# Bucketed attention and two expert layers on one core: where GpSimd's low parts and weight splits and the first head's turn stand in their queues

## What is computed

```python
q_bits = (np.einsum('bhsd,dk->bhsk', q, proj) > 0)      # k_bits alike; bucket = sum(bits * 2**i)
scores = np.where(mask, q @ k.T / sqrt(D), -1e9)
attn = np.exp(scores - max); attn = attn / (sum(attn) + 1e-9)
x = (attn @ v)                                          # 1536 x 512 after the heads are joined
h = x @ w_in1;  g = max(h, 0) + alpha * min(h, 0);      x = g @ w_out1
h = x @ w_in2;  g = P(h) / (Q(|h|) + 1e-6);             out = g @ w_out2
```

## Time and profile before

| what | us |
|---|---|
| median of the 3 runs timed | 798.24 (794.5, 798.24, 799.77) |
| the profiled execution, its own time | 799.15 |
| its span, first to last instruction | 797.3 |
| PE busy in it | 775.7 |
| DVE, ACT, POOL busy | 517.8, 358.3, 304.9 |

### The profile page before, as it was taken

The page is one execution under the profiler, slowest core; times in us unless marked ns, Lnnn a source line. Parts: engine busy times, 40 slices in busy tenths (PEclk is TensorE's granted clock), DMA queues, the critical chain, the costliest instruction groups (busy, mean ns, idle before and its releaser), DMA issues.

```text
span 797.3 us, 11723 instructions
## 1 busy us (share of the span) xinstructions
PE 775.7 (97%) x3820; PEld 583.7 (73%) x3820; DVE 517.8 (65%) x806; ACT 358.3 (45%) x588; POOL 304.9 (38%) x357
## 2 busy tenths in 40 slices
PE   8889999999989999999999999999999999999998
PEld 5456565666656778888888888887888888888886
DVE  6776676776751654435333533379888988888886
ACT  7434554555544311112011210167766767676673
POOL 7566776776856689200000177781000000000000
PEclk9999999999999999999999999999999999999999
DMA  4666675675571243000000033330000100000001
GB/s 127 169 153 161 165 199 151 165 203 150 139 187 48 78 139 122 28 1 1 0 1 14 1 106 93 92 93 1 2 0 1 53 0 1 1 27 27 1 1 53
DMA packets 34207, 58.86 MB, mean 74 GB/s; under 512 B 9900, under 2 KB 13780, under 8 KB 34164
## 3 DMA queue, kind: packets, MB, share of 16 engines
q1 hardware_dynamic: 31796, 53.15, 24.3%
q10 hardware_dynamic: 2368, 5.15, 2.6%
HBM read 29.59 MB, written 3.24 MB: 41 GB/s over the span
## 4 chain that ended last, share of the span: by engine, by line
PE 75%; POOL 8%; issue 4%; DVE 4%; SPq 3%; DMA 3%; ACT 1%; POOLq 0%; DVEq 0%; ACTq 0%
PE acc L1375 31%; PE ps_h L1343 31%; PE ps_o L590 3%; PE ps_a L505 2%; PE ps_s L560 2%; PE ps_s L565 2%; POOL lo L866 1%; PE ps_o L612 1%; POOL p_sum L873 1%; DMA work<-rden_scratch 1%; POOL pen L882 1%; DMA q<-stats 1%; PE ps_a L501 1%; POOL x_lo L964 1%; DMA raw<-in_qk 1%
## 5 line engine op out<-in xcount | busy, mean ns | idle before, releaser
L1408 ACT ACTIVATE g_hi<-num 128x512 fp32r<-128x512 f32 x96 | 59.9, 624 | 207.2 <-PE acc L1375 203.1
L1478 DVE TENSOR_TENSOR g_lo<-num,g_hi 128x512 fp32r<-128x512 f32 x96 | 71.7, 747 | 78.2 <-ACT g_hi L1408 77.7
L1040 DVE TENSOR_REDUCE row_max<-ps_a 128x1 f32<-128x384 f32 x180 | 92.1, 553 | 40.0 <-PE ps_a L505 37.6
L736 ACT ACTIVATE p<-ps_s 128x768 f32<-128x768 f32 x96 | 77.5, 810 | 67.7 <-PE ps_s L565 64.2
L1343 PE MATMUL ps_h<-x_hi,w_late_in_hi 128*128 128x512 f32 x288 | 78.9, 395 | 1.2 <-POOL w_late_in_lo L1307 1.2
L1343 PE MATMUL ps_h<-x_hi,w_late_in_lo 128*128 128x512 f32 x288 | 78.8, 394 | 0.0
L1343 PE MATMUL ps_h<-x_lo,w_late_in_hi 128*128 128x512 f32 x288 | 78.8, 394 | 0.0
L590 PE MATMUL ps_o<-p,v_use 128*64 128x384 f32 x384 | 74.4, 507 | 0.0
L1486 DVE TENSOR_SCALAR num<-ps_h,alpha_sb 128x512 f32<-128x512 f32 x48 | 36.0, 750 | 54.4 <-PE ps_h L1343 53.7
L1416 ACT ACTIVATE den_q<-ps_h,abs_b 128x512 f32<-128x512 f32 x48 | 33.0, 688 | 83.8 <-PE ps_h L1343 77.6
L1343 PEld LDWEIGHTS ps_h<-x_hi,w_late_in_hi 128*128 128x128 f32 x288 | 53.9, 187 | 14.0 <-POOL w_late_in_lo L1307 1.7
(11 more groups left out here) (167 smaller groups left out, 1569.9 us busy)
## 6 DMA issues: line engine op xcount, KB each, us to landing
stage<-in_w_in SPq DMA_DIRECT2D x26, 256.0 KB, 2.7
stage<-in_w_out SPq DMA_DIRECT2D x26, 256.0 KB, 2.7
raw<-in_qk SPq DMA_DIRECT2D x15, 384.0 KB, 3.0
q<-hi SPq DMA_DIRECT2D x30, 192.0 KB
k<-hi SPq DMA_DIRECT2D x30, 192.0 KB
v_raw<-in_v SPq DMA_DIRECT2D x16, 192.0 KB, 3.0
work<-rden_scratch SPq DMA_DIRECT2D x16, 192.0 KB, 3.3
out<-y SPq DMA_DIRECT2D x12, 256.0 KB, 2.5
```

Source lines behind the costliest of these rows:

```text
L736: nc.scalar.activation(halves(p[c][:]), ps_s[c % 2][:, :, 0:HALF], ACT.Exp, scale=float(D) ** -0.5).then_inc(s_exp, 1)
L1040: dve.tensor_reduce(row_max[slot][:, i, c:c + 1], ps_a[:, i, 0:HALF], AX.X, ALU.max).then_inc(s_a_free, 1)
L1408: nc.scalar.activation(g_hi[f % 2][:], num[f % 4][:], ACT.Copy).then_inc(s_ghi, 1)
L1478: dve.tensor_tensor(g_lo[f % 2][:], num[f % 4][:], g_hi[f % 2][:], ALU.subtract).then_inc(s_glo, 1)
```

## The change

Six moves; no instruction is added to or taken from the work. (1) `uses_of`: in the first head the sign products of head 3 ("bits") go behind the turn of head 1 ("m"). (2) PE: the first scores of head 1, which stood ahead of the last row-maximum products and values of chunk 4 of head 0, go behind those values. (3) ACT: in head 0 the high part of head 3 is made in step 3 and no longer in step 4. (4) POOL: `x_low` leaves the end of pairs 1 to 5 and stands behind `row_stats` of the following pair's u = 0; for that, POOL's program writes out pair 1 ahead of its hardware loop. (5) POOL: the weight splits of chunks 0 and 1 go behind the penalty rows and behind `split_qk`. (6) SP: the load of weight chunk 2 (`stage_early(2)`) goes from pair 6's u = 0, where it stood ahead of the row sums' spreading, to its u = 1, behind the low parts.

```diff
--- before.py
+++ after.py
@@ -277,8 +277,8 @@
                 if first_head:
                     return [([("a", 1, 1)], [("a", 1, 2)]),
                             ([("a", 1, 3)], [("a", 1, 4)]),
-                            ([("a", 1, 5)], [("bits", 3, 0)]),
-                            ([("m", 1, 0)], [("a", 2, 0)]),
+                            ([("a", 1, 5)], []),
+                            ([("m", 1, 0)], [("bits", 3, 0), ("a", 2, 0)]),
                             ([("a", 2, 1)], [("a", 2, 2)]),
                             ([("a", 2, 3)], [("a", 2, 4)])]
                 if second_head:
@@ -352,10 +352,11 @@
 
                 return u
 
-            def over_pairs(eng, body):
-
-                body(0, 2)
-                with eng.Fori(1, PAIRS - 2) as j:
+            def over_pairs(eng, body, begin=1):
+
+                for j in range(begin):
+                    body(j, 2)
+                with eng.Fori(begin, PAIRS - 2) as j:
                     body(j, 2)
                 body(PAIRS - 2, 1)
                 body(PAIRS - 1, 0)
@@ -476,10 +477,10 @@
                             fill_b_lo(u, j + 1)
                         if first:
                             stage_early(u)
-                        if left == 1 and u == 0:
-                            stage_early(2)
                         if u == 0 and not first:
                             spread(sp, j - 1)
+                        if left == 1 and u == 1:
+                            stage_early(2)
                         if not left and u == 0:
                             stage_early(3)
 
@@ -665,7 +666,7 @@
                                 t = KC * h + c
                                 if c + 2 < KC:
                                     scores(u, j, c + 2, t + 2)
-                                elif not (final and u == 1):
+                                elif not (final and u == 1 or first and c == 4):
                                     scores(1 - u, j + u, c + 2 - KC, t + 2)
                                 for kind, g, cc in steps[c][0]:
                                     at = (u + g) % 2, j + (u + g) // 2
@@ -685,6 +686,9 @@
                                 due_sums = False
                             for c in range(begin, begin + group):
                                 values(u, h, c, KC * h + c)
+                                if first and c == 4:
+
+                                    scores(1, 0, 0, c + 2)
                             for c in range(begin, begin + group):
                                 for kind, g, cc in steps[c][1]:
                                     at = (u + g) % 2, j + (u + g) // 2
@@ -835,7 +839,7 @@
                                 sums_of(1 - u, j - 1 + u, h - 1)
                             if c == 1 and first and u == 1:
                                 stat_rows(0, 1)
-                            if c == (4 if first and u == 0 else 2) and (left > 1 or (left == 1 and u == 0)):
+                            if c == (3 if first and u == 0 else 2) and (left > 1 or (left == 1 and u == 0)):
                                 split_qk(1 - u, j + 1 + u)
                             if c == (4 if first and u == 0 else 3) and (left > 1 or (left == 1 and u == 0)):
                                 fill_a_hi(1 - u, h + 3)
@@ -990,14 +994,10 @@
                             if not (isinstance(h, int) and h == 0):
                                 v_partial(1 - u, j + u)
                             row_stats(1 - u, h + 1)
-                        if final and u == 0:
+                        if u == 0 and not (isinstance(j, int) and j < 2):
                             x_low(j - 2)
                         if not (first and u == 0):
                             add(1, h)
-                        if first and u == 1:
-                            split_weights(0)
-                        if left == 1 and u == 0:
-                            split_weights(1)
                         if final:
                             split_weights(2 + u)
                         if left > 1 or (left == 1 and u == 0):
@@ -1008,14 +1008,16 @@
                             split_qk(1 - u, j + 1 + u)
                         if first and u == 0:
                             add(1, h)
-                        if u == 1 and left > 1 and not first:
-                            x_low(j - 1)
+                        if first and u == 1:
+                            split_weights(0)
+                        if left == 1 and u == 0:
+                            split_weights(1)
                         if final and u == 0:
                             normalise(j - 1)
                         if final and u == 1:
                             x_low(j - 1)
 
-                over_pairs(pool, pair)
+                over_pairs(pool, pair, 2)
 
             def attention_vector(dve):
                 dve.memset(mcols[1][:, 0:STAT_ROW].bitcast(F32), 0.0)
```

## The result

The changed kernel takes 790.8 us (median of 7 runs, 789.68 to 792.74), the kernel before 798.26 us beside it (794.5 to 799.77); the ratio is 0.9922, 95% interval 0.9901 to 0.9943. So it is faster by 0.8%: 7.5 us between the medians and 6.2 us by the ratio; 5.4 us were forecast. The two profiled executions, 799.15 and 790.8 us, lie 8.35 us apart. Lines have moved: the turn was L516 and is L517, the row-maxima product L505 and L506, POOL's p_sum L873 and L877.

What follows compares the result with a forecast made beforehand. PE, busy 775.7 of 797.3 us, bounds the kernel; only idle and low-clock time can be won. 3.9 + 1.2 + 0 + 1.7 + 1.5 - 1.4 = 6.9, less 1.5, gives 5.4 us: 798.4 to 793.0, range 790.3 to 796.2.

Steps and rivals of the forecast that it cites:

- (c): Turns in u = 0 of pairs 2 to 6: five waits for POOL go; gain 3.86 us, bounds 2.6 and 3.9.
- the 2.06 us: POOL's wait for the exponentials before its p_sum, which x_lo was to fill, with 0.2 us to spare.
- The rival of a hidden gain: x_lo late for the exponentials' sum, turns keep waiting: 2.9 us less gained, 795.9 us; chance 0.06.
- (a): PE's waits in the first two heads, 3.36 us, become 2.2; gain 1.2 us at head 2's turn, bounds 0.6 and 2.6.
- the waits forecast as 0.8, 0.75, 0.35 and 0.3: PE's new waits: head 1's turn, halves of `ps_a`, the next product, row maxima; 2.2 us together.
- Price nothing: ACT's earlier high part in head 0 taken as free; if the cover is gone, it costs 0.83 us.
- (b): Waits near 54 us (1.61) and at head 3's turn (0.93, growing to 2.2): gain 0, bounds -0.5 and +2.5 us.
- It moves with (a) alone: v_raw's transfer for head 3's turn, landed at 57.05, starts after head 2's turn, so only (a) moves it.
- the third rival: v_raw lands early and both waits of (b) go: 2.5 us more than forecast, 790.5 us; chance 0.07.
- (d): Pair 6: stats wait goes, gain 1.7 us, with its half clock 1.5; head 14's turn waits longer, loss 1.4.
- one new fall of 1.5: Longer waits at head 3's and head 14's turns, each about one chance in two of a 1.5 us clock fall.
- The rule on the shared port: Two-input DVE and SBUF-reading GpSimd instructions exclude each other, first to issue goes first; the trace at pair 0's p_sum disagreed.

Runs made afterwards that it cites:

- the one at 799.28 us: Changed kernel with the weight split of pair 0 back ahead of pen and lo; profiled execution of its slower group, 799.28 us; kernel's ratio to before 0.9992.
- the profile at 792.1 us: Changed kernel with the weight split of pair 0 back ahead of pen and lo; profiled execution of its faster group, 792.1 us.

## Why the prediction was right, and where it was not

The median, 790.8 us, lies inside the forecast range, 0.5 us from its lower end and 2.2 us below the forecast of 793.0. The order of the parts was right, and x_low is the largest of them. Part of the hit was luck: between the profiled executions 8.35 us were gained against 5.4, and had the clock not fallen in the second one, it would have been near 789.3 (an estimate, by the 1.5 us below), outside the range.

- **(c) x_low**, forecast 3.9 (2.6 to 3.9), measured 4.8 in the turns (4.2 where it was taken back) and 3.7 to 4.4 in whole runs. The mechanism was right: the turns wait for nothing, and x_lo fits into the 2.06 us. In the turns the size was off above my upper bound: I took the idle time in the rows as the whole cost of a wait, and each has 0.2 us more. The rival of a hidden gain is excluded.
- **(a) the first two heads**, forecast 1.2, measured 1.23 at head 2's turn, with the waits forecast as 0.8, 0.75, 0.35 and 0.3 found as 0.64, 0.89, 0.14 and 0.07. So the waits fell by 1.6 us, from 3.36 to 1.74, and the turn gained 0.4 us less than that; where these went is open. "Price nothing" for ACT was wrong: its edit carries 1.0 us.
- **(b) the split in pair 0**, forecast 0, is the step that failed. "It moves with (a) alone" held for the start of v_raw's transfer, not for its length: 8.0 and 7.9 us in the two kernels with head and split both old, 7.4 with the new split beside the old head, 6.8 to 7.5 in the change and the kernels with both new, 5.4 to 6.6 with the new head beside the old split. Head 3's turn waits 0.35 us, not 2.2. The two old waits (1.61 and 0.93 us) became 0.65 for pen's transfer, which the sum did not have, and 0.35: 1.5 us were gained, inside the bound of 2.5; the third rival (v_raw lands early, 790.5 us) came about in part. DVE's p_sum was short, as forecast (48.77, 1.93 us in place of 3.50). The larger miss is that I summed (a) and (b): the split must move because the new head sends its weights later. Without its move the ratio is 0.9992, with it 0.9922, which is 5.6 us for a part priced at nothing.
- **(d) pair 6**, forecast +1.7 and +1.5 less 1.4 and less one new fall of 1.5, together 0.3; by the experiment it is worth nothing. Each term was found (1.65 us at the turn, 1.2 lost; no stats wait; one fall), but whether they gain or lose hangs on transfers and on the clock, and both differ from one execution to the next. The later load of chunk 2 was hidden, as forecast, but by little: it landed at 235.9, and POOL's split starts at 235.98; with ACT back the split waits 0.15 us for it.
- **The clock.** One fall was forecast and one came in the profiled execution, which is luck as much as judgement: apart from the last microseconds, seven of the 14 profiles have one fall, four none, two two and one three. That a long wait brings one in every second case was too high: head 14's turn waits 1.58 to 1.65 us in eight profiles, and the clock fell behind it in two, the change's and the one at 799.28 us. Of all 24 waits of 1.5 us or more from 27 us on, eight had a fall behind them or at their end. The other six falls had only shorter waits ahead of them, three of them near 34 us, where no wait was over 0.9 us; so the length of a wait alone doesn't tell. The price was right for a short fall, 1.5 us: turn 1 to turn 2 takes 18.07 us with one (x_low back) and 16.56 without (the change). It was too low for the two that began before a wait of 3 us was over (3.08 us in the profile at 799.28 us, 2.95 with the first head back): the half clock stayed for 6.8 us.
- **The rule on the shared port** was called not borne out by the earlier trace rows, and the split of pair 0 back tried it again. In the profile at 792.1 us p_sum was again passed over by lo while it waited behind pen (3.99 us). At 799.28 us p_sum was issued ahead of pen and took 1.20, and pen took 2.17 in place of 1.46; in the change lo was issued first (48.06) and p_sum (48.77) ended 0.8 us behind it. So the first to issue went first in these two, and the one already waiting did not come next in the other.
- **The rest of the sum**: the wait for the late weights shrank from 1.22 to 0.73 us; it was 0.7 to 2.95 us over the kernels here, so these 0.5 us are scatter.

## What to carry to other kernels

Take work out from between a late result and the instruction that waits for it, and put it into a wait of the same engine whose length the trace shows: that gain came in full, here 0.2 us larger per wait than the idle rows say. Before adding up the parts of a reordering, follow each load's issue time through them: an edit that moves a queue can turn another's cover into a stall, and the two must go together. An in-order engine with a small instruction that needs a DMA (here a reciprocal of 0.22 us) can stop everything behind it; check its slack against the longest landing that the trace shows, not the one it happened to get.

## What was not expected of the hardware

A transfer of one size, v's rows for head 3, took 5.4 to 8.0 us from issue to landing over the 14 profiles, and what beside it made the difference was not isolated. The gather of sums took 2.3 to 4.8 us in one and the same kernel, whose times fell into two groups some 5 us apart. In the same kernel a start 0.08 us behind pen or 0.34 us ahead of it made p_sum take 3.99 or 1.20 us. A wait of 2.09 us (the profile at 792.1 us, ended at 54.83) and one of 2.72 us (x_low back, ended at 280.44) were followed by no fall of the clock, one of 1.65 us was, and in two of some 3 us it fell before the wait was over.
